# Down-projection matmuls reordered by token range, one DVE sum moved, weight splits and the first step re-placed

## The reference

```python
kv = einsum('bhsd,bhse->bhde', k, v);  o = einsum('bhsd,bhde->bhse', q, kv)
x = o / sqrt(mean(o * o, -1) + 1e-6) * g_norm          # 2304 x 512 after the heads are joined
h = x @ w_in   (512 x 2048);  g = h * sigmoid(1.702 h);  x = g @ w_out   (2048 x 512)     # layer 1
h = x @ w_in2  (512 x 2048);  g = softplus(h);           out = g @ w_out2 (2048 x 512)    # layer 2
```

## Time and profile before

| | before |
|---|---|
| runs, median | 975.18 us |
| the profiled execution: its own time, its span | 979.29 us, 977.5 us |
| PE busy, its mean granted clock | 848.5 us (87%), 0.955 |
| DVE, ACT, POOL busy | 590.0, 428.1, 227.0 us |

### The profile page before, as it was taken

The page is one execution under the profiler, slowest core; times in us unless marked ns, Lnnn a source line. Parts: engine busy times, 40 slices in busy tenths (PEclk is TensorE's granted clock), DMA queues, the critical chain, the costliest instruction groups (busy, mean ns, idle before and its releaser), DMA issues.

```text
span 977.5 us, 12329 instructions
## 1 busy us (share of the span) xinstructions
PE 848.5 (87%) x4584; PEld 756.4 (77%) x4584; DVE 590.0 (60%) x1024; ACT 428.1 (44%) x815; POOL 227.0 (23%) x261
## 2 busy tenths in 40 slices
PE   6867898959989879989897989977998987899897
PEld 6756888958889868889887878766887876778785
DVE  4654656665655575664576666666666666666663
ACT  4642232233122123122137565655656556665654
POOL 1598666251232141352421100000000000000000
PEclk9997999979999989999899999998999998999998
DMA  9933537232452642554452242231524222432401
GB/s 309 335 126 118 211 145 291 97 151 97 170 228 98 235 163 98 186 231 164 175 191 98 76 150 77 87 119 37 199 75 144 83 76 76 151 139 76 150 2 64
DMA packets 25674, 139.26 MB, mean 142 GB/s; under 512 B 2448, under 2 KB 8208, under 8 KB 18448
## 3 DMA queue, kind: packets, MB, share of 16 engines
q1 hardware_dynamic: 25040, 138.16, 38.6%
q10 hardware_dynamic: 576, 0.33, 0.1%
HBM read 104.40 MB, written 34.08 MB: 142 GB/s over the span
## 4 chain that ended last, share of the span: by engine, by line
PE 43%; DVE 18%; ACT 16%; DMA 8%; issue 8%; POOL 6%; SPq 0%; ACTq 0%; DVEq 0%
PE ps L549 22%; PE ps L594 10%; PE ps L588 7%; DMA w_in_f<-w_in 5%; DVE gs_f L880 5%; PE ps L591 4%; ACT ex L705 4%; ACT fix L707 3%; ACT ex L703 3%; ACT gs L713 3%; DVE gs_f L888 3%; DVE gs L891 2%; DMA kv_in_sb<-k_v 2%; DVE xs L847 2%; DVE xs_f L839 2%
## 5 line engine op out<-in xcount | busy, mean ns | idle before, releaser
L549 PE MATMUL ps<-xs,w_in 128*128 128x384 f32 x2016 | 424.7, 351 | 86.7 <-DVE gs_f L880 73.9
L549 PEld LDWEIGHTS ps<-xs,w_in 128*128 128x128 f32 x2016 | 366.3, 197 | 120.6 <-issue 80.4
L594 PE MATMUL ps<-w_out,gs 128*128 128x512 f32 x864 | 230.5, 405 | 23.3 <-DVE gs L913 23.3
L880 DVE TENSOR_TENSOR gs_f<-ps,gs_f 128x384 f32<-128x384 f32 x240 | 132.9, 554 | 174.2 <-PE ps L549 170.4
L588 PE MATMUL ps<-gs,w_out 128*128 128x512 f32 x576 | 211.2, 399 | 3.1 <-POOL w_out L418 3.1
L594 PEld LDWEIGHTS ps<-w_out,gs 128*128 128x128 f32 x864 | 164.7, 194 | 56.6 <-issue 29.5
L591 PE MATMUL ps<-gs,w_out 128*128 128x256 f32 x576 | 163.6, 284 | 0.0
L588 PEld LDWEIGHTS ps<-gs,w_out 128*128 128x128 f32 x576 | 110.9, 193 | 22.1 <-POOL w_out L418 3.4
L591 PEld LDWEIGHTS ps<-gs,w_out 128*128 128x128 f32 x576 | 111.5, 194 | 0.0
L697 ACT ACTIVATE lg<-gs_f 128x384 f32<-128x384 f32 x72 | 37.1, 523 | 159.2 <-DVE gs_f L880 159.2
L913 DVE TENSOR_TENSOR gs<-gs_f,gs 128x384 fp32r<-128x384 f32 x96 | 54.1, 564 | 84.0 <-ACT gs L713 81.6
(11 more groups left out here) (58 smaller groups left out, 593.3 us busy)
## 6 DMA issues: line engine op xcount, KB each, us to landing
w_in<-w_kept SPq DMA_DIRECT2D x40, 1792.0 KB, 7.3
w_kept<-w_in SPq DMA_DIRECT2D x16, 1792.0 KB, 8.2
kv_in_sb<-k_v SPq DMA_DIRECT2D x16, 512.0 KB, 10.7
w_in_f<-w_in SPq DMA_DIRECT2D x16, 512.0 KB, 8.1
w_out_f<-w_out SPq DMA_DIRECT2D x16, 512.0 KB, 8.8
q_sb<-q_t SPq DMA_DIRECT2D x16, 288.0 KB, 11.1
out<-xy SPq DMA_DIRECT2D x18, 256.0 KB, 7.7
tail_sb<-k_v SPq DMA_DIRECT2D x3, 256.0 KB, 12.8
```

Source lines behind the costliest of these rows:

```text
L549: mm = nc.tensor.matmul(ps[:, bank, 0:HALF], w[:, wp, W_OF[k], cols], xs[:, k, xp, t], start=(new and t == 0 and (wp, xp) == (HI, HI)), st ...
L594: mm = nc.tensor.matmul(ps[:, ACC_BANK + j, 0:DM], g[:, j * P:(j + 1) * P], w, start=new, stop=done)
L880: nc.vector.tensor_tensor(to, bank, other, ALU.add).then_inc(added, 1)
```

## The change

- **Down** issues the matmuls of the first tokens first, over both f, and then those of the rest. In layer 1 that is 24 matmuls of 256 columns (tokens 0 to 255) and then 24 of 512; in layer 2 18 of 512 for tokens 0 to 383 and then 18 for the rest. The first now waits for the split of C21, the one at half of the list for C22, the one at three quarters for C12. `shares` is one list for nearly all steps, with some down matmuls right behind P1.
- **C12's sum** stands ahead of `gate(m, C22)` in layer 1, and ahead of `low_g(m, C21)` and `softplus(m, C22)` in layer 2.
- **The sums' banks** are emptied in two parts, the first tokens' in the first step of a chunk and the rest in the second step; the stores are issued a step later. Some `round_x` stand further behind, after `round_g(m, C11)`.
- **Layer-2 splits** are in steps 9, 11, 13, 17, 19, 21, 25 and 27. The raw weights of one are loaded right behind the store of the one before.
- **First step**: P1 and P6 of step 0 stand in the attention (units 13 and 14), P2 and P7 between the last turns, and `first_product(0)`, U2 and the sigmoid table load move with them. POOL makes the weights of step 1 before five of the seven slots. `w_out` tiles are rotated so that pair 0 lies beside the attention buffers; it is loaded in unit 10 and its high part made by POOL.

```diff
-            if m >= STEPS - 1 and (m - STEPS + 1) % 2 == 0 and m - STEPS + 1 < 2 * STEPS:
-                return STEPS + (m - STEPS + 1) // 2
-            return None
+            return STEPS + SECOND_AT.index(m) if m in SECOND_AT else None
+        SECOND_AT = (9, 11, 13, 17, 19, 21, 25, 27)
...
+        def w_out_tile(pair):
+            return 2 * ((pair + STEPS - 1) % STEPS)
...
-            W_AT = {3: 0, 8: 1, 13: 2}
+            W_AT = {3: 0, 6: 1, 14: 2}
...
+                if u == 10:
+                    load_w_out(0, 0)
+            keep(0)
             sp.wait_ge(turned, UNITS)
-            load_w_out(0, 0)
             load_w_out(1, 0)
-            keep(0)
...
-                if split_at(m) and split_at(m) >= STEPS:
+                if m == STEPS - 1:
+                    load_raw(STEPS)
+                if m in SECOND_AT:
                     keep(split_at(m))
-                if split_at(m + 1) and split_at(m + 1) >= STEPS:
-                    load_raw(split_at(m + 1))
+                    if split_at(m) + 1 < 2 * STEPS:
+                        load_raw(split_at(m) + 1)
...
             x_early(B21)
+            w_all(1)
+            pool.wait_ge(x_raw_made, x_raws(0, T4))
             for slot in X_EARLY[2:]:
-                if slot == T2:
-                    pool.wait_ge(x_raw_made, x_raws(0, T4))
                 x_early(slot)
-            w_all(1)
+            w_out_low(0)
             w_all(2)
-            w_out_low(0)
...
+                if u == UNITS - 3:
+                    product(0, P1)
+                if u == UNITS - 2:
+                    product(0, P6)
...
             def sums_copied(m, narrow, j):
                 if m < PHASE1:
-                    return 3 if j < 2 else 6
-                return (1, 2, 4, 5, 5, 6)[j] if m == PHASE1 else j + 1
+                    return 1 + j // 2 if narrow else 3 + j
+                return (3, 4, 5, 6, 1, 2)[j] if m == PHASE1 else j + 1
...
-                each = down_size(m) // 2
+                each = down_size(m) // 4
                 for i in range(first, last):
-                    f = 1 - i // each
+                    early, f = i < 2 * each, 1 - i // each % 2
...
-                        pe.wait_ge(g_split, TILES * m + C22 + 1)
+                        pe.wait_ge(g_split, TILES * m + C21 + 1)
...
-                    if i == each:
+                    if i == 2 * each:
+                        pe.wait_ge(g_split, TILES * m + C22 + 1)
+                    if i == 3 * each:
                         pe.wait_ge(g_split, TILES * m + C12 + 1)
...
-                part = (0, 4, 6, 13, 14, 19, 24)
-                if m % STEPS == 0:
-                    part = (2, 4, 6, 14, 18, 24, 24)
-                if m % STEPS == 1 and m > 1:
-                    part = (0, 0, 4, 11, 13, 19, 24)
+                part = (3, 5, 7, 13, 14, 19, 24)
                 if m == ALL - 1:
-                    part = (0, 2, 4, 9, 10, 14, 24)
-                return [x * down_size(m - 1) // 24 for x in part]
+                    part = (2, 3, 5, 9, 10, 14, 24)
+                if m - 1 >= PHASE1:
+                    return [x * 3 // 2 for x in part]
+                return [3 * x if x <= 8 else 24 + (x - 8) * 3 // 2 for x in part]
...
+            product(0, P2)
+            turn(UNITS - 2)
+            product(0, P7)
+            turn(UNITS - 1)
+            product(0, P4)
+            product(0, P5)
+            product(0, P3)
...
                 if m > PHASE1:
                     round_g(m - 1, C12)
+                if p == 1 and ci > 0:
+                    copy_sums(ci - 1, first_copies(ci - 1), ACC_BANKS)
...
                 if phase:
                     softplus(m, C21)
-                    low_g(m, C21)
                 else:
                     gate(m, C21)
+                add(m, C12_ADD)
                 if ends:
                     low_x(ci + 1, T2)
-                if not phase:
+                if phase:
+                    low_g(m, C21)
+                    softplus(m, C22)
+                    low_g(m, C22)
+                else:
                     gate(m, C22)
-                add(m, C12_ADD)
                 if ends:
                     low_x(ci + 1, T3)
-                if phase:
-                    softplus(m, C22)
-                    low_g(m, C22)
```

More of the change, by code:

```diff
@@ L266, in tiles_done @@
         def tiles_done(m):
-            return sum(KT if ci < CHUNKS else ACC_BANKS for ci in range(m // STEPS))
+            return sum(2 * KT if ci < CHUNKS else ACC_BANKS for ci in range(m // STEPS))
         def wait_down(engine, m):
@@ L414, in w_out_low @@
                 pair, layer = w_out_of(m)
-                pool.wait_ge(w_out_hi, STEPS * layer + pair + 1)
-                for f in (2 * pair, 2 * pair + 1):
+                t = w_out_tile(pair)
+                if m == 0:
+                    pool.wait_ge(w_out_landed[pair], 16)
+                    nc.gpsimd.tensor_copy(w_out[:, t:t + 2, HI], w_out32[:, t:t + 2, LO]).then_inc(w_out_hi_early, 1)
+                    pool.wait_ge(w_out_hi_early, 1)
+                else:
+                    pool.wait_ge(w_out_hi, STEPS * layer + pair)
+                for f in (t, t + 1):
                     for cols in (slice(0, DM // 2), slice(DM // 2, DM)):
@@ L552, in product @@
                 mm.then_inc(prod_done, 1)
+            kv_product(0)
+            for u in range(UNITS):
+                if u + 1 < UNITS:
+                    kv_product(u + 1)
+                raw_output(u)
+                if u >= TURN_LAG:
+                    turn(u - TURN_LAG)
+                if u == UNITS - 3:
+                    product(0, P1)
+                if u == UNITS - 2:
+                    product(0, P6)
             def down_size(m):
[L555 removed]
@@ L575, in down @@
                         if m == 0:
                             pe.wait_ge(x_made, UNITS)
-                    if i == each:
+                    if i == 2 * each:
+                        pe.wait_ge(g_split, TILES * m + C22 + 1)
+                    if i == 3 * each:
                         pe.wait_ge(g_split, TILES * m + C12 + 1)
-                    if i < each and which == 0 and p == 0 and ci > 0:
-                        pe.wait_ge(acc_copied, acc_copies(ci - 1) + sums_copied(m, j))
+                    if f == 1 and which == 0 and p == 0 and ci > 0:
+                        pe.wait_ge(acc_copied, acc_copies(ci - 1) + sums_copied(m, early, j))
@@ L581, in down @@
                     g = gs[:, m % 2, f, gp]
-                    w = w_out[:, 2 * p + f, wp]
+                    w = w_out[:, w_out_tile(p) + f, wp]
                     new = p == 0 and f == 1 and which == 0
                     done = p == STEPS - 1 and f == 0 and which == 2
-                    if phase == 0:
-                        cols = slice(j * P, (j + 1) * P)
+                    if phase == 1:
+                        mm = nc.tensor.matmul(ps[:, ACC_BANK + j, 0:DM], g[:, j * P:(j + 1) * P], w,
+                                              start=new, stop=done)
+                    elif early:
@@ L587, in down @@
                         half = ps[:, ACC_BANK + KT + j // 2, j % 2 * NARROW:(j % 2 + 1) * NARROW]
-                        nc.tensor.matmul(ps[:, ACC_BANK + j, 0:WIDE], w[:, cols], g[:, 0:WIDE],
-                                         start=new, stop=done)
-                        mm = nc.tensor.matmul(half, w[:, cols], g[:, WIDE:CHUNK], start=new and j % 2 == 0,
+                        mm = nc.tensor.matmul(half, w[:, j * P:(j + 1) * P], g[:, 0:NARROW], start=new and j % 2 == 0,
                                               stop=done, skip_group_check=True)
@@ L615, in _ @@
                     product(m, k)
[L616 to L622, removed]
+                    down(m - 1, came, shares(m)[k])
+                    came = shares(m)[k]
             down(ALL - 1, 0, down_size(ALL - 1))
@@ L667, in _, with first_product @@
             act.wait_ge(consts_in, 48)
+            def first_product(m):
+                act.wait_ge(prod_done, PRODUCTS * m + P1 + 1)
+                if m >= 2:
+                    wait_down(act, m - 2)
+                nc.scalar.copy(hid(m, C21), ps[:, BANK_A, 0:HALF]).then_inc(t1_made, 1)
             for u in range(UNITS + TURN_LAG):
@@ L672, in _ @@
                     square(u)
+                if u == UNITS - 1:
+                    first_product(0)
+                if u == UNITS:
+                    nc.scalar.preload_act_table_set("sigmoid_and_others")
                 if u >= TURN_LAG:
@@ L676, in _ @@
                     root(u)
-            nc.scalar.preload_act_table_set("sigmoid_and_others")
-            def first_product(m):
-                act.wait_ge(prod_done, PRODUCTS * m + P1 + 1)
-                if m >= 2:
-                    wait_down(act, m - 2)
-                nc.scalar.copy(hid(m, C21), ps[:, BANK_A, 0:HALF]).then_inc(t1_made, 1)
             def hidden(m, tile):
@@ L721, in round_w_out @@
```

(20 more changed lines are left out.)

79 lines of the change are left out of this document (35 added, 44 removed).

## The result

The changed kernel takes 886.7 us, the median of four runs (886.62 to 888.36), against 975.52 before on the same chip; the ratio is 0.909, 95% interval 0.907 to 0.911. The prediction was 861 in a range of 845 to 900. The profiled execution took 886.62 with a span of 884.8, so this time it is within 0.1 us of the median.

What follows compares the result with a forecast made beforehand. PE was taken to bound the kernel where nothing holds it, the rest being gaps and low clock. Stretch times summed to 863.1 us, plus 1.8 around the span 864.9 profiled, hence a median of 861; range 845 to 900.

Steps and rivals of the forecast that it cites:

- the narrow loads: Rival for layer 1's down: narrow matmuls in a row show their weight loads, 0.173 us apart, 33 us more, 894; chance 0.07.
- A gapless step and its price: Ordinary steps without PE waits: layer 1 costs 15.56 us from matmul times (measured 15.68), layer 2 15.8.
- Narrow matmuls in a row: Layer 1's down: 24 256-column matmuls in a row still take 0.115 us each, so the reorder costs nothing.
- C12's sum sooner: DVE's C12 sum moved earlier: P1's gap goes in layer 1 (0.5 us in hand) and the 0.48 gap in layer 2.
- Layer 2's circle: Rival: layer 2's P7-to-P7 chain of waits, 15.7 us against PE's 15.8, binds at 0.6 a step, 873; chance 0.09.
- Chunk ends: Steps at chunk ends: 7 and 8 fall from 46.64 to 34.0 us, 31 and 32 from 48.75 to 40.0.
- First step: Start of the kernel: P1 of step 1 at 70.0 us instead of 77.45, the 5.21 wait for POOL gone.
- Step 25's new wait: Step 25: down(24) waits for ACT's late bank copies, 4.5 us; the step takes 22.4 instead of 17.70.
- Step 24: Chunk end like steps 31 and 32, but with a layer-1 step before it: 18.9 us.
- Layer-2 splits: Moved splits: 0.7 us for step 27; SyncE's loads, `keep` and stores block no load that is due.
- From profile to median: Profiled execution taken to stand 0.42% above the median, as before: 864.9 us becomes a median of 861.
- The port: Rival: POOL and DVE lock each other out, making P1 1.0 us late in 14 split steps, 875; chance 0.04.

## Why the prediction held, and where it was wrong

The measured 886.7 lies in the range of 845 to 900, but not in the 846 to 882 that the prediction gave its own account. The range reached past 882 for the sake of the narrow loads, which were not what cost the time; that it held is in part luck. Step by step:

- **A gapless step and its price**: right. In both layers ordinary steps take 15.73 (15.7 and 15.8 forecast).
- **Narrow matmuls in a row**: right. PE in step 12 of the changed kernel:

```profile
250.91 1.23 PE L615 MATMUL ps<-gs,w_out 128*128 128x256 f32 x9
251.97 1.21 PE L555 MATMUL ps<-xs,w_in 128*128 128x384 f32 x6
```

  Nine 256-column matmuls start within 1.06 us, 0.118 each. The load hides behind a 256 as the earlier trace rows had it; the rival at 0.173 is out. "The reorder costs nothing" was a little too much, though: a layer-1 step without a gap takes 15.60 in the old order (steps 2 to 6 with the sum alone, steps 10 to 14 with the splits alone) and 15.73 in the new one, 3 us in 24 steps. Products and narrow matmuls both start 1 to 2 ns further apart; the runs don't show why.
- **C12's sum sooner**: right for the time. The two experiments from either side give 65.8 (alone) and 47.6 us (taken back). They need not agree, as each gap has several waits behind it: with the sum and the first tokens both in place the ordinary steps have no waits left, and taking either out of the changed kernel brings 48 to 53 back (the 53 with the new `shares`). The mechanism in layer 2 was only half told: the sum also starts ACT's C12 work.
- **Layer 2's circle**: no sign of it in steps 33 to 38 (15.73 each). In steps 26 and 27, with POOL beside DVE, P7 starts 0.60 behind the matmul before it instead of 0.23, waiting for U2 behind C12's softplus: there it does bind, for 0.4 of the microsecond that these steps are longer (16.7 and 16.6).
- **Chunk ends**: right to 1 us for each pair but 23 and 24. Steps 31 and 32 take 17.0 and 22.1, with the waits where they were put: from start to start 1.35 for C22's sum, 0.87 for down's C21, 1.24 for U2 and 3.09 for T1 (1.65, 0.5, 1.35 and 3.0 forecast as time lost; 0.2 of each measured figure is there without a wait).
- **First step**: 72.1 and not 70.0. C12's sum ends at 72.0 (68.9 and 1.1 forecast), as C21's gate on DVE meets POOL's long cast (last section). And one reading was wrong. The profile puts the 5.21 of the earlier trace rows down to POOL's L403, and the prediction took it for POOL's work for step 1. In the kernel before, that work was done at 69.97; C12's sum on DVE ended at 77.30 and P1 started at 77.45:

```profile
64.61 5.36 POOL L403 TENSOR_TENSOR w_in<-w_in_f,w_in 128x256 fp32r<-128x256 f32 x7
```
```profile
76.76 0.54 DVE L880 TENSOR_TENSOR gs_f<-ps,gs_f 128x384 f32<-128x384 f32 x1
```

  So P1 waited for the sum here too, behind C22's gate. With the sum alone moved, and POOL's list as before, P1 of step 1 starts at 74.61. What POOL's new list does remove is step 1's wait for w_out's low part (L418: 3.1 us before, 7.0 with the sum alone). No run has the first-step change alone, so its share of the 5.3 us stays open.
- **Step 25's new wait**: right. PE stands 3.61 us for ACT's copy (4.5 forecast):

```profile
491.35 2.05 PE L610 MATMUL ps<-w_out,gs 128*128 128x512 f32 x4 [3.61 <-ACT xy L780]
```

- **Step 24**: 22.5 instead of 18.9. The wait for T1's low part was 4.37 and not the 3.0 forecast for step 32, since POOL runs beside DVE's work for it (the raw sum takes 1.49 us instead of 0.95), and PE ran part of the step at the low clock (0.85 on average, against 0.92 in step 32):

```profile
478.68 0.69 PE L555 MATMUL ps<-xs,w_in 128*128 128x384 f32 x1 [4.37 <-DVE xs L877]
```

- **The queue: the step that failed.** Under "Layer-2 splits" the prediction said that loads, `keep` and stores "are issued where they don't block a load that is due". I had checked `keep` and the operand loads, and not what the added wait for `keep`'s landing holds up in SyncE's list: the layer-2 w_out load of steps 18, 20 and 22. Its cost is 23.7 us, by the run with the load moved ahead; with it the kernel takes 863.0, against 861 predicted for a kernel in which it did not happen, and PE's wait for DVE's sums is 7.8 us instead of 24.7. The 863.0 is nearer than its parts: the start is 2.7 us longer than forecast, steps 23 to 25 2.3 longer, steps 9 to 22 2.8 and steps 33 to 46 2.7 shorter.
- **From profile to median**: the profiled execution before stood 0.42% above its median, and I took that over (3.6 us). For the changed kernel the two are equal. That offset was the scatter of one execution and not a property to carry over. The 21.7 us of the span and these 3.6 or so make up the miss of 25.7.
- **The port**: see below. The rival's time (875) needed a gap in each split step, and there is none in steps 9 to 17.

## What to carry over

When a wait is added to a queue, list what is issued behind it and who needs that next, and go through it to the engine that waits in order; a wait for a landing in SyncE's list (12.7 us here) held back every load behind it. A gap that one engine's sum seems to cause can be lifted by the order of work on a second engine and by giving PE other work, and what each is worth depends on whether the other is in place (the sum: 65.8 us alone, 47.6 taken back). The engine that a profile names behind a wait is an inference: the end times of everything the instruction waits for decide, as at the start of step 1. Costing steps one by one from measured durations came to 1 us here for six of the ten stretches, so it is worth doing for queues too.

## What the runs showed of the hardware

DVE beside POOL, end of step 0 of the changed kernel:

```profile
68.40 1.89 POOL L418 CAST w_in<-w_in_f 128x1792 fp32r<-128x1792 f32 x1
```
```profile
68.79 1.72 DVE L922 CAST gs<-gs_f 128x384 fp32r<-128x384 f32 x1
```

DVE's cast takes 0.36 us alone (at 345.14). It takes 0.77 in most meetings with POOL, where about 0.55 of a POOL operation is left to run when it begins, and 1.72 here, where 1.50 of a POOL cast of 1.89 are left. In the changed kernel's trace 29 of these casts begin while a POOL operation runs, with 0.48 to 1.50 us of it left, and each ends 0.21 to 0.22 us after that operation.

The Trainium skill (SBUF — State Buffer, section SBUF: two separate sides) calls the port pair that the two engines share an exclusive lock: what starts first has it for its whole instruction, and the other fully blocks. The trace agrees: DVE waits for the rest of the POOL operation that it meets. The 0.4 that I read from the mean was not a weaker rule but the rest of a short operation. So what a POOL operation costs DVE grows with how much of it is left, and a long one can cost more.
